# Folding the last two head pairs together, and moving four sums on GpSimd, ahead of the first channel MLP

## What is computed

```python
# attention with random features, 4 batches x 8 heads x 576 tokens x 64
proj = q_or_k @ w_phi;  proj -= max(abs(proj));  phi = concat(exp(proj), exp(-proj))
x = (phi(q) @ (phi(k).T @ v)) / (phi(q) @ sum(phi(k)) + 1e-6)     # x: 4 x 576 x 512
# first mixer
u = x + real(fft2(x))                    # over tokens and channels
un = (u - mean(u)) / sqrt(var(u) + 1e-6)
x = u + relu(un @ w_ch1) @ w_ch2         # 512 -> 2048 -> 512: the first channel MLP
# second mixer
u = x + token_mlp(x);  out = u + relu(u @ w1) @ w2
```

## Time and profile before

| | before |
|---|---|
| median of three runs | 968.9 us |
| the profiled execution | 972.43 us, of which its span 970.6 us |
| TensorE busy | 957.7 us, 99% of the span |
| VectorE busy | 471.9 us, 49% |
| ScalarE busy | 325.7 us, 34% |
| GpSimd busy | 188.2 us, 19% |

### The profile page before, as it was taken

One profiled execution on the slowest core, in us unless ns is written; L12 is line 12 of the kernel. 1 busy time (PEld: TensorE's weight loads), 2 busy tenths in 40 slices (PEclk: granted clock), 3 DMA queues, 4 the chain that ended last, 5 costly groups with the idle time before them and its releaser, 6 DMA issues.

```text
span 970.6 us, 17962 instructions
## 1 busy us (share of the span) xinstructions
PE 957.7 (99%) x7523; PEld 862.5 (89%) x7523; DVE 471.9 (49%) x939; ACT 325.7 (34%) x650; POOL 188.2 (19%) x163
## 2 busy tenths in 40 slices
PE   8999999999999999999999999998999999999998
PEld 6999999979999999899999999887999899999997
DVE  6998888861421322222313213453684544635543
ACT  6886857744311111211111112253432212213211
POOL 3654746389500000000000000037000000000000
PEclk9999999999999999999999999999999999999999
DMA  7242333335210020010010110578220020200101
GB/s 235 78 116 60 104 100 101 118 127 173 93 66 1 1 66 1 1 65 0 24 41 0 58 56 25 193 268 291 75 87 1 7 83 1 87 1 1 44 1 44
DMA packets 50032, 70.16 MB, mean 72 GB/s; under 512 B 22948, under 2 KB 23976, under 8 KB 49832
## 3 DMA queue, kind: packets, MB, share of 16 engines
q1 hardware_dynamic: 48232, 62.84, 20.1%
q10 hardware_dynamic: 1728, 6.29, 1.8%
HBM read 50.24 MB, written 18.87 MB: 71 GB/s over the span
## 4 chain that ended last, share of the span: by engine, by line
PE 75%; DMA 1%; POOL 1%; DVE 0%; ACT 0%; issue 0%; POOLq 0%
PE mlp_y L1196 7%; PE mlp_y L1197 7%; PE mlp_hid L1183 7%; PE mlp_hid L1181 7%; PE mlp_hid L1182 7%; PE mlp_y L1195 7%; PE mlp_y L1643 5%; PE mlp_y L1644 5%; PE mlp_y L1645 5%; PE mlp_hid L1630 2%; PE mlp_hid L1631 2%; PE mlp_hid L1632 2%; PE mlp_turn L1632 2%; PE mlp_turn L1631 2%; PE mlp_turn L1630 2%; DMA mlp_w_raw<-in_w_mlp 1%
## 5 line engine op out<-in xcount | busy, mean ns | idle before, releaser
L1314 DVE SCALAR_TENSOR_TENSOR mlp_h_lo<-mlp_hid,mlp_h_hi 128x384 fp32r<-128x384 f32 x96 | 53.5, 557 | 258.1 <-ACT mlp_h_hi L1231 258.1
L1231 ACT ACTIVATE mlp_h_hi<-mlp_hid 128x384 fp32r<-128x384 f32 x96 | 47.2, 492 | 284.0 <-PE mlp_hid L1183 284.0
L1181 PE MATMUL mlp_hid<-mlp_ut_hi,mlp_w_hi 128*128 128x384 f32 x384 | 130.7, 340 | 0.0
L1183 PE MATMUL mlp_hid<-mlp_ut_hi,mlp_w_lo 128*128 128x384 f32 x384 | 129.4, 337 | 0.0
L1182 PE MATMUL mlp_hid<-mlp_ut_lo,mlp_w_hi 128*128 128x384 f32 x384 | 128.8, 336 | 0.0
L1195 PE MATMUL mlp_y<-mlp_w_hi,mlp_h_hi 128*128 128x512 f32 x288 | 113.1, 393 | 1.8 <-DVE mlp_h_lo L1314 1.8
L1197 PE MATMUL mlp_y<-mlp_w_hi,mlp_h_lo 128*128 128x512 f32 x288 | 114.6, 398 | 0.0
L1196 PE MATMUL mlp_y<-mlp_w_lo,mlp_h_hi 128*128 128x512 f32 x288 | 114.3, 397 | 0.0
L1564 POOL TENSOR_TENSOR mlp_w_lo<-mlp_w_raw,mlp_w_hi 128x1024 fp32r<-128x1024 f32 x12 | 28.4, 2395 | 393.5 <-DVE tok_x_lo L2052 381.4
L1643 PE MATMUL mlp_y<-mlp_w_hi,mlp_h_hi 128*128 128x512 f32 x216 | 84.5, 391 | 1.6 <-DVE mlp_h_lo L1838 1.6
L1644 PE MATMUL mlp_y<-mlp_w_lo,mlp_h_hi 128*128 128x512 f32 x216 | 84.4, 391 | 0.0
(11 more groups left out here) (219 smaller groups left out, 2136.6 us busy)
## 6 DMA issues: line engine op xcount, KB each, us to landing
mlp_w_raw<-in_w_mlp SPq DMA_DIRECT2D x14, 512.0 KB, 4.1
mlp_w_raw<-in_w_mlp ACTq DMA_DIRECT2D x12, 512.0 KB, 6.7
v<-in_v SPq DMA_DIRECT2D x16, 320.0 KB, 3.6
qk<-in_kT SPq DMA_DIRECT2D x16, 288.0 KB, 4.0
mlp_u<-u_scratch SPq DMA_DIRECT2D x6, 768.0 KB, 4.6
qk<-in_qT SPq DMA_DIRECT2D x15, 288.0 KB, 4.0
u_scratch<-x_all SPq DMA_DIRECT2D x4, 1024.0 KB, 4.7
mlp_u<-u_scratch SPq DMA_DIRECT2D x4, 1024.0 KB, 5.6
```

The lines of the kernel that those rows point to most:

```text
L1181: nc.tensor.matmul(out, w_hi[:, j, col], hi, start=(c == 0), stop=False)
L1183: last = nc.tensor.matmul(out, w_lo[:, nf - 1 - j, col], hi, start=False, stop=(c == DC - 1))
L1231: nc.scalar.activation(h_hi[:, j % 2, :], hid[j % 2][:, 0:BT], ACT.Relu).then_inc(h_rounded, 1)
L1314: nc.vector.scalar_tensor_tensor(out=h_lo[:, j % 2, :], in0=hid[j % 2][:, 0:BT], scalar=0.0, in1=h_hi[:, j % 2, :], op0=ALU.max, op1=ALU.s ...
```

## The change

The tile sum and column fold of pair 14 are no longer made ahead of the last division. One function on each engine makes them for pairs 14 and 15 together: 256 columns of three tiles (768 elements a partition), then 255 mirrored columns (765). GpSimd makes the difference of the one row that `edge` needs first (1x256), then the edge, and only then the whole difference. The first `pool_add` goes ahead of the wait for `normed`; weight chunk 2 goes right behind the last fold, ahead of `pool_add(LAST - 1, 1)`, and the wait for `fold_split` 8 ahead of it is gone. ScalarE rounds weight chunk 2 ahead of the folds.

```diff
@@ scalar_beside
         if j == 1:
+            mlp1["act_weights"](act, [2])
             act_fold(act, LAST, 0)
             act_third(act, LAST, 0)
             act_edge(act, LAST)
             act_fold(act, LAST, 1)
             act_third(act, LAST, 1)
-            mlp1["act_weights"](act, [2])
@@ VectorE
-    def dve_last_sum(dve):
-
-        cols = slice(D - 2 * DH, D)
+    def dve_last_folds(dve):
+
         dve.wait_ge(x_done, PAIRS)
-        dve.wait_ge(odd_folded, 2 * B - 1)
+        dve.wait_ge(tail_done, len(TAIL_ON_ACT))
         x = x_of(LAST)
-        nc.vector.tensor_tensor(fold_s[:, :, cols], x[:, 0:FRONT, cols], x[:, 5:2:-1, cols],
-                                ALU.add).then_inc(summed, 1)
-
-    def dve_last_even(dve):
-
-        low, high = MIRROR[1]
+        nc.vector.tensor_tensor(fold_s[:, :, LAST_TWO], x[:, 0:FRONT, LAST_TWO], x[:, 5:2:-1, LAST_TWO],
+                                ALU.add).then_inc(summed, 2)
+        low, high = MIRROR_BOTH
         dve.wait_ge(summed, PAIRS)
         nc.vector.tensor_tensor(fold_s[:, :, low], fold_s[:, :, low], fold_s[:, :, high],
-                                ALU.add).then_inc(even_folded, 1)
+                                ALU.add).then_inc(even_folded, 2)
@@ dve_step
-            if s == 4 and k == PAIRS - 1:
-                dve_fold(dve, Pair(k - 1))
@@ vector
-        dve_last_sum(dve)
+        dve_last_folds(dve)
@@ vector_beside
-        if j == 0:
-            dve_last_even(dve)
@@ GpSimd
-    def pool_last_fold(pool):
-
-        cols = slice(D - 2 * DH, D)
+    def pool_last_folds(pool):
+
+        x, tile = x_of(LAST), TILE_OF[0]
+        o = fold_d[0:1, tile]
         pool.wait_ge(x_done, PAIRS)
-        pool.wait_ge(odd_folded, 2 * B - 1)
-        x = x_of(LAST)
-        nc.gpsimd.tensor_tensor(fold_d[:, :, cols], x[:, 0:FRONT, cols], x[:, 5:2:-1, cols],
-                                ALU.subtract).then_inc(differed, 1)
-        low, high = MIRROR[1]
-        o = fold_d[0:1, TILE_OF[0]]
-        pool.wait_ge(differed, PAIRS)
+        nc.gpsimd.tensor_tensor(o[:, LAST_TWO], x[0:1, tile, LAST_TWO], x[0:1, 5 - tile, LAST_TWO],
+                                ALU.subtract).then_inc(row_differed, 1)
+        low, high = MIRROR_BOTH
+        pool.wait_ge(row_differed, 1)
         pool.wait_ge(even_folded, 2 * B)
         nc.gpsimd.tensor_copy(edge[:, 0:257:256], o[:, 0:257:256])
-        nc.gpsimd.tensor_tensor(edge[:, low], o[:, low], o[:, high], ALU.add).then_inc(edge_made, 1)
+        nc.gpsimd.tensor_tensor(edge[:, low], o[:, low], o[:, high], ALU.add).then_inc(edge_made, 2)
         pool.wait_ge(edge_made, 2 * B)
+        nc.gpsimd.tensor_tensor(fold_d[:, :, LAST_TWO], x[:, 0:FRONT, LAST_TWO], x[:, 5:2:-1, LAST_TWO],
+                                ALU.subtract).then_inc(differed, 2)
+        pool.wait_ge(differed, PAIRS)
         nc.gpsimd.tensor_tensor(fold_d[:, :, low], fold_d[:, :, low], fold_d[:, :, high],
-                                ALU.subtract).then_inc(odd_folded, 1)
+                                ALU.subtract).then_inc(odd_folded, 2)
@@ pool_step
         if k == PAIRS - 1:
+            pool_add(pool, LAST - 1, 0)
             pool.wait_ge(*mlp1["first_normed"])
             mlp1["gpsimd"](pool, (), 0, 2)
-            pool_add(pool, LAST - 1, 0)
@@
-        for n in (k - 2, k - 1) if k % 4 == 2 and 6 <= k else () if k % 4 == 1 and 5 <= k else ready(k):
+        for n in (k - 2, k - 1) if k % 4 == 2 and 6 <= k else () if k % 4 == 1 and 5 <= k or k == PAIRS - 1 else ready(k):
@@ gpsimd
-        pool_last_fold(pool)
+        pool_last_folds(pool)
+        mlp1["gpsimd"](pool, (), 2, 3)
         pool_add(pool, LAST - 1, 1)
-        pool.wait_ge(fold_split, 2 * B)
-        mlp1["gpsimd"](pool, (), 2, 3)
         pool_add(pool, LAST - 1, 2)
```

More of the change, by code:

```diff
@@ L177, in front @@
     differed = sem("differed")
+    row_differed = sem("row_differed")
     even_folded = sem("even_folded")
@@ L215, in front @@
     MIRROR = [(slice(129, 256), slice(383, 256, -1)), (slice(1, 129), slice(511, 383, -1))]
+    MIRROR_BOTH = (slice(1, 256), slice(511, 256, -1))
+    LAST_TWO = slice(D - 4 * DH, D)
     THIRD = [slice(TCOLS // 3 * i, TCOLS // 3 * (i + 1)) for i in range(3)]
```

## The result

The changed kernel takes 975.19 us (median of four runs, 974.51 to 976.36) against 969.05 us of the kernel before in the same comparison. The ratio is 1.0055, with a 95% interval of 1.0040 to 1.0071. The forecast was 973.3 us and slower; the range was 969.0 to 976.0. Its profiled execution took 975.65 us, with a span of 973.8 us.

The account below looks back on a forecast made before the run. TensorE, 99% busy, bounds the kernel, so only its idling and clock could change. Terms +1.8 + 0.9 + 1.2 = +3.9 us on the profiled 972.43 us; carried over to the 968.9 us median: 973.3 us, range 969.0 to 976.0.

Parts of the forecast that it names:

- Part 1: First `pool_add` ahead of `normed`: four of VectorE's nine 1/sqrt steps each wait for a GpSimd sum, +1.8 us.
- The slip that I allowed for: At TensorE's third turning of the rows: no more than 0.1 us of the 1/sqrt delay is lost.
- Part 2: Folds behind the last division: TensorE's idling ahead of the second product falls from 1.85 to 1.0 us, -0.85 us.
- Part 3: Fold split: `dve_edge` waits for GpSimd's chunk 2; s2 starts at 209.5 against 208.63, +0.9 us together with the earlier folds.
- Part 4: TensorE's clock: new idling in s0, ahead of s2 and at the turning brings one or two falls, +1.2 us.
- ScalarE's chunk 2: Rounding chunk 2 ahead of the folds takes ScalarE 1.05 us before a fold VectorE couldn't take up anyway: nothing.
- The rival of blocking in part: Small steps slip between GpSimd's sums or `dve_edge` precedes chunk 2; s2 at 208.1 to 209.5, 970.4 us; chance 0.20.
- the two small marks: Prediction wrong if VectorE's nine 1/sqrt steps still take 1.7 us in all, or `dve_edge` (L776) ends before chunk 2 begins.

Follow-up runs that it names:

- a_adds_back: Changed kernel with the first `pool_add` put back behind weight chunks 0 and 1: 971.83 us, ratio 1.0023.
- a_chunk2_back: Changed kernel with GpSimd's weight chunk 2 put back behind the second `pool_add` and its wait for `fold_split` 8: 971.00 us, ratio 1.0012.
- a_both_back: Changed kernel with both GpSimd moves undone (first `pool_add` and weight chunk 2 put back): 970.85 us, ratio 1.0007.
- the repeated execution: The kernel before, unchanged, profiled for a second trace: 968.56 us, against 972.43 us for the first.
- b_chunk2_ahead: Kernel before with GpSimd's weight chunk 2 right behind the last fold, without the wait for `fold_split` 8: 969.54 us, ratio 0.9989.
- b_adds_rstd: Kernel before with the first `pool_add` ahead of `normed` but behind the last of the nine 1/sqrt steps: 969.83 us, ratio 0.9984.
- a_both_back_row_late: Changed kernel with both GpSimd moves undone and the odd row's difference made behind the even fold: 970.07 us, ratio 1.0000.

## Why the prediction was right, and where its sizes were off

- **Part 1, +1.8 us.** Measured 1.89 us, shown by `a_adds_back` and, on the other kernel, `a_chunk2_back` against `a_both_back`. The mechanism was the one given: four steps wait for four sums. The slip that I allowed for, some 0.1 us, was not there.
- **Part 2, -0.85 us ahead of the second product.** The gap is 1.32 us and not 1.0: -0.5. The term mis-sized is the sum beside the row's difference. I had put 0.4 us for the blocking, on both folds together; the sum alone lost 0.58 (1.54 against 0.96). The rest is two gaps of 0.1 us that I had left out, ahead of the sum and behind it.
- **Part 3, s2 at 209.5 plus the shift of 1.8.** Measured 211.69, forecast 211.3. `dve_edge` waited for chunk 2 as described. Against a kernel before without the fall of the clock, parts 2 and 3 were to cost 209.5 - 207.55 = 1.95 us and cost 2.2 (4.12 - 1.9).
- **Part 4, the clock, +1.2 us.** One fall, 1.1 us, in the trace of after; by their mean clocks (0.998, 0.996, 0.996, 0.998) its four runs had one or two, as forecast. It was also right that the first trace of before had a fall that costs 1.1 to 1.2 us, and that other runs have none. The two stretches of idling at the turning (1.17 and 0.57 us) brought none.
- **The level.** The forecast was +4.4 us on the median, and +6.1 came; the measured time lies near the upper end of the range. Against the first trace of before, which it was added up on, the sum of +3.9 us fits: +4.0 at `hid` of chunk 2 (5.23 - 1.21). What was off is the way from there to the median. The sum is 1.8 + 1.95 + 1.2 = 4.95 us against a run without the fall, 973.9; measured at `hid` of chunk 2: 5.23. The median came out at 975.2, 1.3 above that. In the trace of after 1.7 us are added at the second entrance, by a landing of 8.68 us. The prediction didn't know of that place: it put what the first execution had above the median to the profiler and the clock, and 2.6 us of it arose at this landing. That the profiler costs anything no run shows; the repeated execution was profiled too and took 968.56 us. Whether the landings of all four runs of after were late, and whether a shift of the earlier part makes them so, is open: the repeated kernel shows that it varies by itself, and ten runs of `a_chunk2_back`, 2.4 us late, have a median of 971.0.
- **ScalarE's chunk 2, costed at nothing.** It delays nothing by itself, but by `b_chunk2_ahead` it is the condition under which GpSimd's chunk could come in front of `dve_edge`. Part 3 put the chunk right behind the odd fold and so leaned on this edit without saying it; no term of the sum is wrong by it.
- **The rival of blocking in part** would have had s2 at most at 209.5; the two small marks named for the prediction being wrong (nine steps of 1.7 us, L776 ahead of chunk 2) didn't occur.

## What to carry to other kernels

An idle stretch of GpSimd isn't free space as long as VectorE works on operands in SBUF: ask of each operation moved into it which VectorE operations lie beside it, however small, and who waits for them. A wait that seems to have no reason, such as the one for `fold_split` ahead of chunk 2, may be what keeps a long GpSimd operation off a short one of VectorE; where the long one must go there, cut it. When single runs differ by more than the edit is worth, compare traces at one and the same instruction rather than totals.

## What the hardware showed that I had not expected

- The scaling of three tiles with one tensor input in SBUF took 2.80 us beside GpSimd's sums and 1.46 us alone (`b_adds_rstd`).
- A GpSimd operation on a single partition (1x256, 0.73 us) stretched a 128-partition sum of VectorE from 0.96 to 1.54 us (`a_both_back_row_late`).
- The granted clock fell behind an idle stretch of 1.85 us in one execution of the kernel before and not in another with 1.83 us. A fall costs 1.1 to 1.2 us by the time of `hid` of chunk 2. Runs of the kernel before with a mean clock of 1.0 have a median of 968.7 us, those at 0.998 of 970.2, the two at 0.993 took 975.6.
- The landing that ends the wait at the second MLP's entrance took 7.01 and 9.50 us in two executions of one kernel.
